# Routing of the first 18 token groups inside the last two slots of a one-core attention, MLP and MoE kernel

## The reference

```python
def _attn_ref(q, k, v, a_re, a_im):                 # 4 batches, 8 heads, 768 steps, 48 wide
    mag = np.sqrt(a_re * a_re + a_im * a_im)
    scale = np.minimum(mag, 0.999) / (mag + 1e-06)
    a_re_n, a_im_n = (a_re * scale, a_im * scale)
    for t in range(S):
...
        kv = np.einsum('bhd,bhe->bhde', k[:, :, t], v[:, :, t])
        S_re, S_im = (ar * S_re - ai * S_im + kv, ar * S_im + ai * S_re)
        y[:, :, t] = np.einsum('bhd,bhde->bhe', q[:, :, t], S_re)
...
def _moe_ref(x, w_in, w_out):                       # 384 -> 2048 -> 384
    h = x @ w_in
    sp = np.where(h > 20.0, h, np.log1p(np.exp(np.minimum(h, 20.0))))
    g = h * np.tanh(sp)
    return (g @ w_out).astype(np.float32)
...
def _moe2_ref(x, modality_id, w_gate, modality_bias, w1, w2):   # 8 experts, 384 -> 1024 -> 384
    logits = x @ w_gate + modality_bias[modality_id]
    e_idx = np.argmax(logits, axis=1)
    probs = np.exp(logits - logits.max(-1, keepdims=True))
    probs /= probs.sum(-1, keepdims=True) + 1e-09
    gate_w = probs[np.arange(N), e_idx]
    for e in range(E):
        mask = e_idx == e
        h = np.maximum(x[mask] @ w1[e], 0.0)
        out[mask] = gate_w[mask, None] * (h @ w2[e])
```

## Time and profile before

| | |
|---|---|
| time, median of 3 runs | 1044.2 us (1041.66 to 1046.25) |
| the profiled execution | 1047.15 us, of which the span of its records is 1045.4 |
| PE busy | 967.3 us, 93% |
| DVE busy | 710.5 us, 68% |
| ACT busy | 574.1 us, 55% |
| POOL busy | 91.1 us, 9% |
| granted TensorE clock, mean | 0.965 of full |

### The profile page before, as it was taken

How to read it: one execution, slowest core, us unless ns; L and a number is a source line. 1 busy time by engine, 2 the same in 40 slices (tenths; PEclk the granted TensorE clock), 3 DMA queues, 4 the chain that set the end, 5 groups by cost and what they waited for, 6 DMA issues and landing times.

```text
span 1045.4 us, 18746 instructions
## 1 busy us (share of the span) xinstructions
PE 967.3 (93%) x6522; PEld 936.2 (90%) x6523; DVE 710.5 (68%) x1286; ACT 574.1 (55%) x1068; POOL 91.1 (9%) x150
## 2 busy tenths in 40 slices
PE   5879899999999999999999999994389999999996
PEld 3769798999999999999999999994389999999996
DVE  4646998988888988888888866876543333653432
ACT  6557886876776876777776764551013223222221
POOL 2000000000000000000000000000022222342221
PEclk9898999999999999999999999997689999999998
DMA  9702111121121121121121110000251111441110
GB/s 210 213 2 32 39 30 32 39 62 39 39 61 39 39 61 39 39 61 39 39 62 39 24 31 1 1 24 25 84 191 42 38 38 45 154 147 38 38 44 24
DMA packets 146259, 58.65 MB, mean 56 GB/s; under 512 B 131353, under 2 KB 140583, under 8 KB 146192
## 3 DMA queue, kind: packets, MB, share of 16 engines
q1 hardware_dynamic: 139056, 42.61, 17.2%
q0 software_dynamic: 3936, 10.44, 3.2%
q10 hardware_dynamic: 3200, 4.72, 1.2%
HBM read 48.21 MB, written 10.03 MB: 56 GB/s over the span
## 4 chain that ended last, share of the span: by engine, by line
PE 86%; DVE 5%; ACT 3%; DMA 3%; issue 2%; POOL 0%; SPq 0%; POOLq 0%; DVEq 0%; ACTq 0%
PE bank L1566 20%; PE bank L1547 19%; PE bank L1764 12%; PE bank L1775 11%; PE bank L1473 4%; PE bank L1512 4%; PE bank L1460 4%; PE bank L1514 3%; PE bank L1495 3%; DMA w_sb<-in_moe_w_dram 2%; PE bank L1417 1%; PE bank L1410 1%; PE bank L1747 1%; PE bank L1738 1%; PE bank L1584 1%
## 5 line engine op out<-in xcount | busy, mean ns | idle before, releaser
L1764 PE MATMUL bank<-xg_t,w_sb 128*128 128x128 f32 x1296 | 150.5, 277 | 1.3 <-DVE xg_t L1371 1.3
L1764 PEld LDWEIGHTS bank<-xg_t,w_sb 128*128 128x128 f32 x1296 | 149.8, 193 | 1.7 <-issue 1.7
L1547 PE MATMUL bank<-x_hi,w_in_hi 128*128 128x384 f32 x384 | 141.4, 368 | 1.2 <-DVE x_lo L1070 1.2
L1566 PE MATMUL bank<-w_out_hi,g_hi 128*128 128x392 f32 x384 | 141.2, 368 | 0.0
L1547 PE MATMUL bank<-x_hi,w_in_lo 128*128 128x384 f32 x384 | 130.9, 341 | 0.0
L1547 PE MATMUL bank<-x_lo,w_in_hi 128*128 128x384 f32 x384 | 130.9, 341 | 0.0
L1566 PE MATMUL bank<-w_out_hi,g_lo 128*128 128x392 f32 x384 | 130.7, 340 | 0.0
L1566 PE MATMUL bank<-w_out_lo,g_hi 128*128 128x392 f32 x384 | 130.7, 340 | 0.0
L929 ACT ACTIVATE he<-bank 128x128 f32<-128x128 f32 x216 | 59.8, 277 | 114.9 <-PE bank L1764 111.5
L751 ACT ACTIVATE hid<-bank 128x384 f32<-128x384 f32 x128 | 62.2, 486 | 84.4 <-PE bank L1547 83.6
L933 ACT ACTIVATE o_sb<-bank,gate_now 128x384 f32<-128x384 f32 x27 | 15.7, 581 | 124.7 <-PE bank L1775 124.7
(11 more groups left out here) (279 smaller groups left out, 2089.8 us busy)
## 6 DMA issues: line engine op xcount, KB each, us to landing
w_sb<-in_moe_w_dram SPq DMA_DIRECT2D x8, 1536.0 KB, 6.8
ab<-in_a_re_dram SPq DMA_DIRECT2D x24, 192.0 KB, 2.9
ab<-in_a_im_dram SPq DMA_DIRECT2D x24, 192.0 KB, 3.2
x_rows<-x_sb ACTq DMA_DIRECT2D x8, 576.0 KB, 3.3
qk_raw<-in_q_dram SPq DMA_DIRECT2D x22, 192.0 KB, 3.3
qk_raw<-in_k_dram SPq DMA_DIRECT2D x22, 192.0 KB, 3.4
v_in<-in_v_dram SPq DMA_DIRECT2D x22, 192.0 KB, 2.8
w_out_sb<-in_moe_w_out_dram SPq DMA_DIRECT2D x4, 768.0 KB, 6.1
```

The source lines that it names most:

```text
L1547: last = mm(bank_h[f % 2][:, 0:TT], w[:, kk, f * P:(f + 1) * P], x[:, m % 2, kk], start=(kk == 0 and i == 0), stop=(kk == KD - 1 and i == 2))
L1566: last = mm(bank_x2[t][:, 0:DE], g[:, u % RING, f % QF, t * P:(t + 1) * P], w[:, f], start=(f == 0 and i == 0), stop=(f == FT - 1 and i == 2))
L1764: last = mm(bank_h[f % 2][:, 0:P], w1_sb[par][:, kk, f * P:(f + 1) * P], xg_t[:, kk], start=(kk == 0), stop=(kk == KD - 1))
```

## The change

**Routing.** The bias of all 24 groups (`route_bias`), the choice for the first 18 groups (`choose`) and their running counts (`count_early`) are emitted on DVE in gaps 21, 25 and 28 of slot 6. In slot 7 PE takes the ranks of the 18 groups behind gap 1 (`early_ranks`), and DVE turns them into places (gap 4, `place_ranks`), gates (gap 6) and three quarters of `in_lo` in two pieces of nine groups (gaps 8 and 10, `low_places`). The last six groups go through the same functions behind the last slot. A place within an expert is now split into tile and column before the first tile of the expert is added, to the tile alone. `in_hi` and `carried` are made in two halves of 12 groups, and the ordering product has 66 columns and waits for each half apart. The routing's buffers lie in memory that the slots have done with, so some wait on `x2_out` or `y_ready`; the wait for `x2_out` on DVE now stands before the copy of the order.

**Loads.** SP no longer waits for the first gather before it loads w2.

**Start.** The scales of chunk 3 are taken on ACT ahead of the angle work, and their logarithms are summed into `bank_h[1]` right behind `key_values(2)`. The carry of chunk 4 goes: its turns are summed by a product more, of the angles of chunk 3 with `all_turns`. The fresh rows stand in `cs` and not in `ee`.

```diff
-    RUN_AT = NG.bit_length() % 2
+    GE = (NT - 2) * G3
+    GL = NG - GE
+    EARLY_AT, LATE_AT = GE.bit_length() % 2, GL.bit_length() % 2
+    BIAS_AT, CHOOSE_AT, COUNT_AT = 21, 25, 28
+    RANK_AT, GATE_AT, LO_AT = 4, 6, (8, 10)
+    GH = NG // 2
...
-                    sp.wait_ge(gathered, 16)
...
-            first_carry(FIRST)
...
+                    if m == NT - 1 and g == 0:
+                        act.wait_ge(shifted, 1)
+                        act.activation(work[:, 0:GE], work[:, 0:GE], ACT.Exp).then_inc(exped, 1)
...
             log_mag(4)
+            scales(3)
             attend(0, 9)
             angles_next()
             turn_angle(3)
...
-            scales(3)
...
+            act.wait_ge(shifted, 2)
+            act.activation(work[:, GE:], work[:, GE:], ACT.Exp).then_inc(exped, 1)
...
+                    if m == NT - 2 and g == BIAS_AT:
+                        route_bias(straight)
+                    if m == NT - 2 and g == CHOOSE_AT:
+                        dve.wait_ge(x2_copied, 2 * GE)
+                        choose(straight, 0, GE, shifted)
+                    if m == NT - 2 and g == COUNT_AT:
+                        count_early(straight, chosen_ready)
+                    if m == NT - 1 and g == RANK_AT:
+                        dve.wait_ge(ranks_ready, 1)
+                        place_ranks(straight, bank_a, 0, GE)
+                    if m == NT - 1 and g == GATE_AT:
+                        dve.wait_ge(exped, 1)
+                        gates(straight, 0, GE)
+                    if m == NT - 1 and g in LO_AT:
+                        dve.wait_ge(y_ready, NCH)
+                        n = LO_AT.index(g)
+                        low_places(straight, GE // 2 * n, GE // 2 * (n + 1))
...
+            def route_bias(then):
...
+                for mod in range(NM):
+                    then(dve.tensor_scalar(total[:], mod_f[:], float(mod), None, ALU.is_equal))
+                    then(dve.tensor_tensor((work if mod else bias_all)[:], over_e(total, 0, NG),
+                                           bias_rows[:, mod:mod + 1].to_broadcast([P, NG, E]), ALU.mult))
+                    if mod:
+                        then(dve.tensor_tensor(bias_all[:], bias_all[:], work[:], ALU.add))
+                then(dve.tensor_tensor(up_to_e[:], iota_e[:].rearrange("p (a e) -> p a e", a=1).to_broadcast([P, E, E]),
+                                       iota_e[:].rearrange("p (e a) -> p e a", a=1).to_broadcast([P, E, E]), ALU.is_ge))
+            def choose(then, a, b, ready):
...
+                then(dve.tensor_tensor(biased[:, a:b], logits[:, a:b], bias_all[:, a:b], ALU.add))
+                then(dve.tensor_reduce(best[:, a:b], biased[:, a:b], AX_X, ALU.max))
+                dve.tensor_tensor(work[:, a:b], biased[:, a:b], over_e(best, a, b), ALU.subtract).then_inc(ready, 1)
+                then(dve.tensor_tensor(chosen[:, a:b], biased[:, a:b], over_e(best, a, b), ALU.is_equal))
+                then(dve.tensor_tensor(chosen[:, a:b], chosen[:, a:b], rank_e, ALU.mult))
+                then(dve.tensor_reduce(total[:, a:b], chosen[:, a:b], AX_X, ALU.max))
+                then(dve.tensor_tensor(chosen[:, a:b], rank_e, over_e(total, a, b), ALU.is_equal))
+            def sum_up(then, sides, n, at_end, ready):
...
+                while sh < n:
+                    then(dve.tensor_copy(sides[1 - side][:, 0:sh], sides[side][:, 0:sh]))
+                    last = dve.tensor_tensor(sides[1 - side][:, sh:], sides[side][:, sh:], sides[side][:, 0:n - sh], ALU.add)
+                    if 2 * sh < n:
+                        then(last)
...
+                last.then_inc(ready, 1)
+            def count_early(then, ready):
+                then(dve.memset(running[0][:, 0], 0.0))
+                then(dve.tensor_copy(running[0][:, 1:], chosen[:, 0:GE]))
+                sum_up(then, running, GE + 1, EARLY_AT, ready)
+            def place_ranks(then, bank_, a, b):
+                then(dve.tensor_tensor(biased[:, a:b], bank_[:, 0:(b - a) * E].rearrange("p (g e) -> p g e", e=E), chosen[:, a:b],
...
+                then(dve.tensor_reduce(total[:, a:b], biased[:, a:b], AX_X, ALU.add))
...
+                then(dve.tensor_copy(slot_lo[:, a:b], part_i[:, a:b]))
+                then(dve.tensor_scalar(part_i[:, a:b], slot_i[:, a:b], P.bit_length() - 1, None, ALU.arith_shift_right))
+                then(dve.tensor_copy(slot_hi[:, a:b], part_i[:, a:b]))
+            def gates(then, a, b):
+                then(dve.tensor_reduce(gate[:, a:b], work[:, a:b], AX_X, ALU.add))
+                then(dve.tensor_scalar(gate[:, a:b], gate[:, a:b], 1e-9, None, ALU.add))
+                then(dve.reciprocal(gate[:, a:b], gate[:, a:b]))
+            def low_places(then, a, b):
+                then(dve.tensor_tensor(in_lo[:, a:b], iota_lo[:].rearrange("p (a n) -> p a n", a=1).to_broadcast([P, b - a, P]),
+                                       slot_lo[:, a:b].rearrange("p (g a) -> p g a", a=1).to_broadcast([P, b - a, P]), ALU.is_equal))
...
-            add_carry(4)
...
             dve.wait_ge(x2_copied, 2 * G3 * NT)
...
-            dve.wait_ge(x2_out, 16 * NT)
...
+            choose(straight, GE, NG, shifted)
+            dve.wait_ge(chosen_ready, 1)
+            straight(dve.tensor_copy(late_run[0][:, 0], running[EARLY_AT][:, GE]))
+            straight(dve.tensor_copy(late_run[0][:, 1:], chosen[:, GE:]))
+            sum_up(straight, late_run, GL + 1, LATE_AT, chosen_ready)
+            dve.wait_ge(exped, 2)
+            gates(straight, GE, NG)
+            dve.wait_ge(ranks_ready, 2)
+            straight(dve.tensor_copy(count[:], bank_b[:, GL * E:GL * E + E]))
...
             def up_to(x, out_):
...
+                straight(dve.tensor_tensor(of_run_x[:], up_to_e[:], x.rearrange("p (a e) -> p a e", a=1).to_broadcast([P, E, E]),
+                                           ALU.mult))
+                straight(dve.tensor_reduce(out_, of_run_x[:], AX_X, ALU.add))
             up_to(count[:], ends[:])
             straight(dve.tensor_tensor(first[:], ends[:], count[:], ALU.subtract))
...
+            place_ranks(straight, bank_b, GE, NG)
+            low_places(straight, GE, NG)
             first_e = first[:].rearrange("p (a e) -> p a e", a=1).to_broadcast([P, NG, E])
...
+            straight(dve.tensor_tensor(biased[:], chosen[:], first_e, ALU.mult))
             straight(dve.tensor_reduce(dest[:], biased[:], AX_X, ALU.add))
...
+            straight(dve.tensor_tensor(slot_hi[:], slot_hi[:], dest[:], ALU.add))
+            for half in range(2):
+                gs = slice(half * GH, (half + 1) * GH)
+                def over_columns(t):
+                    return t[:, gs].rearrange("p (g a) -> p g a", a=1).to_broadcast([P, GH, GC])
+                straight(dve.tensor_tensor(in_hi[:, gs], iota_hi[:].rearrange("p (a n) -> p a n", a=1).to_broadcast([P, GH, GC]),
+                                           over_columns(slot_hi), ALU.is_equal))
+                dve.tensor_tensor(carried[:, gs, 0], in_hi[:, gs], over_columns(iota_tok), ALU.mult).then_inc(dest_ready, 1)
+                dve.tensor_tensor(carried[:, gs, 1], in_hi[:, gs], over_columns(gate), ALU.mult).then_inc(dest_ready, 1)
             straight(dve.tensor_copy(runs_f[:, TOTALS, 0:1], ends[:, E - 1:E]))
+            straight(dve.tensor_scalar(active[:], count[:], 1.0, None, ALU.min))
             up_to(active[:], ends[:])
             straight(dve.tensor_tensor(ends[:], ends[:], active[:], ALU.mult))
             straight(dve.tensor_scalar(ends[:], ends[:], 1.0, None, ALU.subtract))
...
             straight(dve.tensor_copy(runs_i[:], runs_f[:]))
             dve.tensor_scalar(runs_i[:, TOTALS, 1:2], runs_i[:, TOTALS, 1:2], 1, None, ALU.arith_shift_right
                               ).then_inc(runs_ready, 1)
+            dve.wait_ge(x2_out, 16 * NT)
...
-                if x % NC:
+                if x % NC and x != FIRST + 1:
...
-                mm(bank_b[:, 0:DM], turn_sum[:], angle_of(x), start=True, stop=True).then_inc(turns_summed, 1)
+                last = mm(bank_b[:, 0:DM], turn_sum[:], angle_of(x), start=True, stop=x != FIRST + 1)
+                if x == FIRST + 1:
+                    last = mm(bank_b[:, 0:DM], all_turns[:], angle_of(FIRST), start=False, stop=True)
+                last.then_inc(turns_summed, 1)
...
+            def early_ranks(known, ready):
+                pe.wait_ge(known, 1)
+                mm(bank_a[:, 0:GE * E], earlier[:], chosen[:, 0:GE].rearrange("p g e -> p (g e)"), start=True, stop=False)
+                mm(bank_a[:, 0:GE * E], ones[:], running[EARLY_AT][:, 0:GE].rearrange("p g e -> p (g e)"), start=False, stop=True
+                   ).then_inc(ready, 1)
...
+                    if m == NT - 1 and g == 1:
+                        early_ranks(chosen_ready, ranks_ready)
...
+            fourth_logs()
...
+            pe.wait_ge(chosen_ready, 2)
+            run = late_run[LATE_AT]
```

(7 more changed lines are left out.)

## The result

| | before | after |
|---|---|---|
| median, first comparison | 1044.34 us (4 runs) | 1036.74 us (4 runs, 1035.99 to 1038.43) |
| ratio, 95% interval | | 0.9937 [0.9912, 0.9962] |
| median, second comparison, made later | 1044.96 us (14 runs) | 1035.81 us (6 runs, 1032.13 to 1040.44) |
| ratio, 95% interval | | 0.9915 [0.9886, 0.9945] |
| the profiled execution | 1047.15 us, span 1045.4 | 1036.13 us, span 1034.4 |

The change makes the kernel 7.6 us faster by the medians of the first comparison, 9.2 by those of the second. Forecast were 16.4 us, 1028, with a range up to 1036. The sign was right; the gain forecast was about twice the measured one. A ratio is formed from all runs and not from the two medians, so it can stand about a microsecond off their difference.

What follows compares the result with a forecast made beforehand. PE bounds the slots; behind 717 us a chain of routing, ordering product, gather and w2 load does. Gains 12.7 + 2.9 + 4.5 less 0.55 and 3.1 give 16.4 us: profile 1047.15 to 1030.7, median 1028, range 1022 to 1036.

Steps and rivals of the forecast that it cites:

- The ordering product: PE, routing behind the slots: 24 products of 66 columns take 6.6 us, at most the 7.17 of before.
- between the routing and w2: From DVE's first routing instruction to the first w2 product: 37.7 us in place of 50.4, a gain of 12.7.
- The start of the ordering product: Behind the slots: PE may start it 11.4 us behind DVE's first routing instruction, before 22.4.
- the table of runs: DVE, behind the second half of `in_hi` and `carried`: ready at 17.5 us, before 27.86.
- What ends the wait for w2: First run: the load, landed at 31.6 us, sets the first w2 product at 37.7; at the far end the gather does.
- the gather's branch: First run: gather starts at 21.3 us, takes about 5.5; w1's last product ends 9.6 behind landing, at 35.6 to 39.3.
- The clock in front of the w2 products: PE's gap before w2 falls under 1 us and the clock holds: gain 2.9 us, other end 0.
- The last slot: Hidden product of f = 9: late DVE work delays ACT's copy; 3.1 us lost (0 to 4), 1.6 more if the clock falls.
- The ranks product: Gap 1 of the last slot, new on a full PE: 0.55 us lost (0.4 to 0.9).
- The start: Near 75 us: chunk 3's scales earlier and chunk 4's carry gone; gain 4.5 us (2 to 5.5), which stays.
- The slower rival: Last slot becomes DVE's, the 4.5 us delay paid in each of five later units: 1047 to 1050 us, chance 0.07.

Runs made afterwards that it cites:

- experiment 2: The changed kernel with the ordering product 128 columns wide again in place of 66; 1031.93 us, ratio to before 0.9876.
- experiment 3: The kernel before with only its ordering product made 66 columns wide; 1046.43 us, ratio to before 1.0019.
- experiment 6: The changed kernel, gates and `in_lo` moved behind DVE's last unit, product narrow, 18, 26 and 34 unread products added in TensorE's tail waits; 1025.92 us, ratio 0.9841.
- experiment 8: The changed kernel with SP's wait for the first gather ahead of the load of w2 restored; 1035.59 us.
- experiment 5: The changed kernel with gates and `in_lo` moved behind DVE's last unit and the ordering product 128 columns wide; 1027.19 us, ratio to before 0.9848.
- experiment 12: The kernel of experiment 8 run once more, beside the changed kernel on the same chip; 1038.67 us.
- experiment 10: The kernel of experiment 5 with SP's wait for the first gather ahead of the load of w2 restored; 1031.49 us against 1027.19.
- experiment 7: The kernel before with only the change's part in the start; 1040.76 us, ratio to before 0.9974.
- experiment 9: The kernel of experiment 6 with 44 added products in place of 34 and 7 more behind the first transposes; 1026.57 us, ratio to before 0.9844.
- experiment 11: The changed kernel, unaltered, run and profiled once more on the same chip as experiment 12; 1035.81 us.

## Why the prediction was too high

- **The ordering product, the step that failed.** The prediction said that 24 products of 66 columns take 6.6 us and that "more than today's 7.17 they can't be". They took 10.52. With them 3.9 us shorter the first w2 product would have come after 38.0 us and not 41.9, so 3.9 of the 4.2 us missing between the routing and w2 are this term. The bound took the clock's rise in the wider product for granted. The durations at one level were nearer: at the upper level 5.57 us (predicted 5.0), at the lower 10.52 (0.39 us a product predicted, 0.44 measured). (3 us at the lower level and the rest at the upper give 6.4 and not 6.6.) That it is the width and not the history is shown by experiments 2 and 3, one in each kernel; why the width matters to the clock stays open.
- **The start of the ordering product** was put at 11.4 us behind the first routing instruction; it came at 11.8. The count of DVE steps held, and so did the table of runs, ended at 17.8 for 17.5.
- **What ends the wait for w2.** The prediction said the load, whose branch doesn't run through the ordering product. The load came when it should: the share of the DMA engines is 1.01 in the microsecond up to 749 and 0.08 in the next, so both loads had landed some 30.7 us behind the first routing instruction (31.6 predicted). The late product made it the gather: it started at 25.3 us and not 21.3, took 6.28 us for the 5.5 predicted, and 10.4 us passed from its landing to the w2 product (9.6 taken from before). With an ordering product of 6.6 us the gather's branch would have come to 38.0 us beside the 37.7 by the load, so its own errors would have cost 0.3 us, or 1.5 with the 7.49 us of experiment 6. What is queued behind w1 does count for the gather: 6.28 us with w2 there, 3.21 without in experiment 8, at the same distance from w1.
- **The clock in front of the w2 products** was up, 3.0 us gained for the 2.9 forecast. It had been at 0.50 since the ordering product and rose within the w1 products, at about 756 us; PE then went on to w2 without a pause, where before it stood 3.35 us.
- **The last slot.** The stall was forecast to 0.1 us, with its place and its cause. The 1.6 us that a fallen clock adds was named and left out of the sum; it fell in four of five traces and cost 1.2 to 2.5 us (38.41 us for the 37.26 of experiment 2 in this one). The ranks product cost what was taken: PE would have reached f = 9 at 675.51, 3.25 us before the 678.76 of before, and the start had given 3.91, so 0.66 us went for a term of 0.55.
- **The start** gave 3.9 for 4.5 in the trace, and alone 4.5 in the trace and 3.4 by the medians.
- **The runs' own spread.** 16.4 less 5.4 is the 11.0 of the profiles. The medians show 7.6 and 9.2, because the profiled execution of before was 2.8 us above its median and that of after 0.6 below. So 3.4 of the 8.8 us between 16.4 and 7.6 are no error of the sum. The prediction took the whole difference of the profiles off the median as well, and no run shows which of its terms were smaller in a median execution of before. The range ended 0.7 us below the first median; the second, 1035.81, lies in it.
- The slower rival, a last slot that becomes DVE's, did not come: one stall, and the backlog wore off.

## What to carry to other kernels

A product that is made narrower is costed from rows at the clock level that it will run at, and a rise of the clock that a wider product saw is not carried over to it: under 128 columns the clock rose 3.3 to 5.9 us into the product, under 66 it had not after 10.5. Work moved under a busy engine is best put where its own engine is idle in the trace, not where there is slack on average: 3.6 us of DVE's work cost 3.0 to 5.5 us in the middle of the last slot and nothing at its end. And when a load is issued earlier, look at the small transfer beside it that becomes the next link.

## What the hardware showed that was not expected

- The same 24 products, 66 or 128 columns wide, with PE and PEld busy all through: 66 wide, TensorE stayed at 1.2 GHz for all of 10.52 us, in six traces; 128 wide, it rose to 2.4 GHz in all six, 3.3 us into the product in the kernel before, 3.7 in experiment 5 and 5.9 in experiment 2, whose windows of one us show 0.50 to 734 and 0.99 behind it. Why the rise comes at such different times with the same width is open.
- At 1.2 GHz a pass of 66 columns costs the same 0.2 us as one of 128, and at 2.4 GHz both cost 0.11 to 0.12.
- The gather of 128 rows took 3.10 to 3.24 us when the load of w1 was through or nearly so (experiments 3, 8 and 12, started 5.2 to 6.0 us behind the issue of w1), and 4.18 to 5.02 beside w1 alone, the more, the sooner it followed (3.1 us behind w1 in experiment 10, 2.2 in experiment 7). Beside both loads it took 6.02 to 6.46. Beside both from their start it took 7.49 in experiment 6, and in experiment 9 at most 6.6, since PE turned its rows at 740.57, that long behind its start at 733.97.
- A stall of 3.0 us of TensorE in full work was followed by a fallen clock in four executions of the same code (0.50 for some 3.5 us in the first profile of the changed kernel and near 7 in experiment 11) and not in the fifth (experiment 2).
